# A fused attention, gated mixing and Fourier kernel: inner tiles of the second transform added by VectorE, and three steps moved by a slot

## The chip, the cores and the metric

One Trainium2 chip, one of its cores. The metric is the device time of one execution in microseconds (us); lower is better. All arithmetic is float32, or float32 split into a rounded high part and a low part (fp32r), so that a product takes three matmuls.

## The reference

```python
# attention, per batch (4) and head (8), seq 576, head_dim 64
scores = scale * np.matmul(q, k.transpose(0, 1, 3, 2))
thresh = np.max(scores, axis=-1, keepdims=True) - tau
scores = np.where(scores >= thresh, scores, -1000000000.0)
attn = softmax(scores); out = np.matmul(attn, v)
# gated mixing, x is (4, 576, 512)
xk = mu_k * x + (1.0 - mu_k) * x_prev;  xr = mu_r * x + (1.0 - mu_r) * x_prev
k = np.maximum(xk @ w_k, 0.0);  v = k * k @ w_v;  r = sigmoid(xr @ w_r);  x = r * v
# Fourier mixing, then a normalised MLP (512 -> 2048 -> 512)
mixed = np.real(fft(fft(x, axis=1), axis=2));  u = x + mixed
un = (u - mean) / np.sqrt(var + 1e-06)
out = u + np.maximum(un @ w_ch1, 0.0) @ w_ch2
```

## The kernel before, in words

Each engine runs a list of its own, written out by hand; only semaphores tie the lists together. The lists are built from a common table of **slots**. Slot n handles query tile n of the attention: there are 36 tiles in a batch (4 pairs of heads, 9 tiles in a pair) and 144 in all. Beside the attention of batch b+1 runs the dense work of batch b, placed by slot numbers counted from the start of batch b+1. "Slot 7" below means slot 7 of such a batch.

In a slot the engines do, in this order:
- TensorE (PE): `qk(n)` scores of tile n; `transpose_probs(n-3)`; `pv(n-4)`; then the dense work of the slot.
- VectorE (DVE): `row_max(n)` (L1249) which reads the scores from PSUM; `mask(n-1)` (L1263); then the dense work, the older batch's first. From the second batch on the scores have one PSUM buffer, so `qk(n)` waits until `row_max(n-1)` is done (L731).
- ScalarE (ACT): `exp(n)` (L998, L999); dense work; `copy_units(n-2)` (L1008) copies transposed probabilities out of PSUM; `copy_head(n-5)` (L1021, L1026) copies a finished head from PSUM to `x_att`, in slots where a head ended.
- GpSimd (POOL): `split_step` (L541 to L563) splits keys and queries of a coming head into high and low parts: step 1 `k_hi`, step 2 the high part of `q_hl`, step 3 `k_lo`, step 4 the low part of `q_hl`; the first steps of a pair are spread over three slots by `second_head` and `next_head` (steps 3 and 4 in one slot). Then the dense work.
- SyncE (SP) issues the DMAs.

The dense work of a batch, by slot: x, the transposes of `x_att` (L845, L850) at 2, 2, 4, 5, 5 (`X_AT`), copied out by DVE and ACT (L1336, L1090); mixing, 16 steps at `MIX_AT`: ACT scales `xT` (L1070), DVE adds (L1282), ACT rounds to `mix_h` one slot later (L1084), POOL subtracts to `mix_l` in that slot (L614); then the matmul groups "r" (slots 8 to 11, four groups; the first needs `mix_l` of steps 0 to 3), "k" and "v" from slot 12 on by `slot_of`; the first "k" group needs `mix_l` of steps 4 to 7. Then the two transforms: fold, "y", and "u". The five u groups stand at slots 39, 39, 42, 42, 43 (`U_AT`), so in slots 3, 3, 6, 6, 7 of the next batch. From u groups 0 to 3 ACT and DVE form `diff[0..1]` and `summ[0..1]` (L1147, L1396, L1397), and POOL adds them into the four tiles of `x2T` (`add_dft`, L645 and L646, two instructions a tile): tile 0 in slot 6, tiles 1 and 2 in slot 7, tile 3 in slot 8, after ACT copied one row of u group 4 (L1153, L1154). The sum is stored by DMA (L465). Mixing step 4 rounds into memory that the adds still read, so ACT waits for all of them (L1078).

In the last batch (from slot 144 on) there is no attention beside the dense work. After it comes the MLP, five chunks of columns.

Of the kernel before, what the change touches and what calls it, by code (L numbers as in the profile page):

```python
# [92 lines left out]
X_AT = [2, 2, 4, 5, 5]  # L93
MIX_AT = [3, 4, 5, 6, 7, 8, 9, 10, 12, 13, 14, 15, 17, 18, 19, 20]
FOLD_AT = [32, 35]
# [10 lines left out]
def alone(d):  # L106
    return d == B - 1
# [6 lines left out]
def slot_of(d, stage, c, i, part=0):  # L114

    if (stage, c) == ("r", 0):
        return 8 + i
    done = 0
    for other in stages(d)[1:]:
        if other == (stage, c):  # L120
            return 12 + (done + i * PARTS[stage] + part) * 23 // 36
        done += GROUPS[other[0]] * PARTS[other[0]]
# [42 lines left out]
def build(nc, qT, kT, v, tau, mu_k, mu_r, w_k, w_v, w_r, w_1, w_2, dft_d, dft_odd, dft_s, ident_in, cd_scr, odd_scr, cs_scr, u_scr, out):  # L165
    ctx = ExitStack()
    with ctx:
# [205 lines left out]
        head0_k_hi, head0_q_hi, head0_first, head0_k_low, qk_hi, k_rounded = [sem(n) for n in ("head0_k_hi", "head0_q_hi", "head0_first", "head0_k_low", "qk_hi", "k_rounded")]  # L373
        k_split, qk_split, v_padded = sem("k_split"), sem("qk_split"), sem("v_padded")
        scores_ready, max_ready, thr_ready = sem("scores_ready"), sem("max_ready"), sem("thr_ready")
# [37 lines left out]
        with nc.Block() as block:  # L413

            @block.sync
            def _(sp):
# [35 lines left out]
                def store_u(d):  # L452
                    if d == B - 1:
                        yield X_AT[4] + 1
                        sp.wait_ge(tx_ready, B * 5)
                        load_u(0, 0)
                        load_u(1, 1)
                        load_w2(0)
                    yield U_AT[4] + 2
                    if d == B - 1:  # L460
                        load_w2(1)
                        sp.wait_ge(dft_ready, B * 5)
                        load_w2(2)
                    sp.wait_ge(u_part, d * 3 + 3)
                    sp.dma_start(u_scr[:, :, d * S:d * S + S], x2T[:, :, :]).then_inc(u_stored, 16)  # L465
# [69 lines left out]
            def _(pool):  # L535
# [7 lines left out]
                def split_step(pair, p, step):  # L543
                    n = pair * 2 + p
                    if step == 1:
                        pool.wait_ge(qk_in[p], 64 * pair + 64)
                        if pair > 0:

                            pool.wait_ge(scores_ready, pair * TILES_PAIR if p else pair * TILES_PAIR - FULL)
                        rounded(k_hi[:, p, :], k_raw[:, p, :]).then_inc(k_rounded, 1)  # L550
                    if step == 2:
                        rounded(q_hl[:, p, :], q_raw[:, p, :]).then_inc(qk_hi, 1)
                    if step == 3:
                        pool.wait_ge(k_rounded, n)
                        nc.gpsimd.tensor_tensor(k_lo[:, p, :], k_raw[:, p, :], k_hi[:, p, :].bitcast(F32), ALU.subtract).then_inc(k_split, 1)
                    if step == 4:
                        if n == 1:

                            pool.wait_ge(qk_split, 1)

                        pool.wait_ge(k_split, n)
                        pool.wait_ge(qk_hi, n)
                        nc.gpsimd.tensor_tensor(q_hl[64:128, p, :], q_raw[64:128, p, :], q_hl[64:128, p, :].bitcast(F32), ALU.subtract).then_inc(qk_split, 1)  # L563
                        pool.wait_ge(qk_split, n + 1)

# [50 lines left out]
                def dense(d):  # L616
# [374 lines left out]
            def _(act):  # L991
# [65 lines left out]
                def mixing(d):  # L1057

                    for i in range(16):
# [26 lines left out]
                def dense(d):  # L1086
# [134 lines left out]
            def _(dve):  # L1221
# [108 lines left out]
                def dense(d):  # L1330
# [61 lines left out]
                    for pr in range(2):  # L1392
# [143 lines left out]
```

## Time and profile before

| what | value |
|---|---|
| runs | 1119.99 us median of 3 (1119.54 to 1124.38) |
| profiled execution | 1123.25 us |
| its span, first to last instruction | 1121.4 us |
| mean granted TensorE clock | 0.983 |
| busy share PE, DVE, ACT, POOL | 96%, 50%, 46%, 37% |
| MLP, by the span | from about 711 us to the end |

Read the table as one engine that is nearly always busy and three that are not: PE's idle time over the whole span is some 41 us, and the profiled execution is 3.3 us longer than the median run.

### The profile page before, as it was taken

To read this page: it belongs to the slowest core of one execution; us is meant where nothing else is said; L and a number is where in the kernel's file an instruction comes from. 1 tells how busy PE (TensorE), PEld (TensorE's weight loads), DVE (VectorE), ACT (ScalarE), POOL (GpSimd) and SP (SyncE) were. 2 spreads that over 40 slices of the span, in tenths; PEclk is the share of its full clock that TensorE was granted. 3 is DMA by queue.
4 is the path that set the end of the run, shared out by engine and by line. 5 is a ranking of instruction groups with operands and counts; after the bars stand their busy time and mean duration, and the time that the engine had idled before them with its cause. 6 is when DMAs were issued, how large, how long until landed. Compare 5 with 4: busy or idle time off the path is not lost.

```text
span 1121.4 us, 18463 instructions
## 1 busy us (share of the span) xinstructions
PE 1080.7 (96%) x7088; PEld 1013.4 (90%) x7088; DVE 557.5 (50%) x1081; ACT 513.2 (46%) x1250; POOL 419.5 (37%) x360
## 2 busy tenths in 40 slices
PE   6999999999999999899998997999999999999998
PEld 6989999998899998899996996888888888888998
DVE  6998764565564565564562557344214214123211
ACT  4989875646775646776643733221111011011110
POOL 3897663533763533762512364350111111111000
PEclk9999999999999999999997997999999999999999
DMA  8635111041211141301112107300200200100000
GB/s 229 181 98 169 41 39 34 26 145 45 88 34 34 32 141 42 95 26 34 39 65 105 44 1 289 117 1 1 68 1 1 68 1 1 67 1 1 35 1 33
DMA packets 37251, 69.30 MB, mean 62 GB/s; under 512 B 4134, under 2 KB 18604, under 8 KB 36140
## 3 DMA queue, kind: packets, MB, share of 16 engines
q1 hardware_dynamic: 36860, 67.80, 19.1%
q8 instruction: 56, 0.92, 0.4%
q10 hardware_dynamic: 304, 0.33, 0.1%
q14 instruction: 31, 0.25, 0.1%
HBM read 55.84 MB, written 12.28 MB: 61 GB/s over the span
## 4 chain that ended last, share of the span: by engine, by line
PE 81%; DVE 7%; POOL 5%; issue 3%; ACT 3%; DMA 0%; ACTq 0%; DVEq 0%; POOLq 0%
PE PB L714 20%; PE PB L716 19%; PE PB L715 19%; PE PB L771 9%; PE PB L741 6%; PE PB L754 5%; DVE probs L1263 2%; DVE neg_s L1249 1%; POOL mix_l L614 1%; POOL x2T L645 1%; POOL q_hl L563 1%; POOL fold_l L637 1%; ACT exps L999 1%; POOL x2T L646 1%; DVE pair_sum L1406 1%
## 5 line engine op out<-in xcount | busy, mean ns | idle before, releaser
L1207 ACT ACTIVATE h_hi<-PB 128x464 fp32r<-128x464 f32 (+1 forms) x80 | 44.5, 556 | 335.6 <-PE PB L716 335.6
L1438 DVE SCALAR_TENSOR_TENSOR h_lo<-PB,h_hi 128x464 fp32r<-128x464 f32 (+1 forms) x80 | 51.0, 638 | 264.0 <-ACT h_hi L1207 264.0
L771 PE MATMUL PB<-v_sb,probsT 128*128 128x64 f32 (+1 forms) x1440 | 178.7, 272 | 0.0
L771 PEld LDWEIGHTS PB<-v_sb,probsT 128*128 128x128 f32 x1440 | 173.7, 193 | 0.0
L1008 ACT ACTIVATE probsT<-PB 128x384 f32<-128x384 f32 (+1 forms) x288 | 109.6, 433 | 83.7 <-PE PB L754 82.7
L1263 DVE SCALAR_TENSOR_TENSOR probs<-neg_s,thresh,exps 128x576 f32<-128x576 f32 x144 | 146.7, 1019 | 0.2 <-PE PB L754 0.2
L1249 DVE TENSOR_SCALAR_CACHE_REDUCE neg_s<-PB,taus 128x576 f32<-128x576 f32 x144 | 117.1, 813 | 39.6 <-PE PB L741 35.2
L714 PE MATMUL PB<-un_h,w1h 128*128 128x464 f32 (+1 forms) x320 | 121.7, 380 | 0.0
L716 PE MATMUL PB<-un_h,w1l 128*128 128x464 f32 (+1 forms) x320 | 118.9, 371 | 0.0
L715 PE MATMUL PB<-h_lo,w2h 128*128 128x464 f32 (+1 forms) x320 | 118.8, 371 | 0.0
L714 PE MATMUL PB<-h_hi,w2h 128*128 128x464 f32 (+1 forms) x320 | 118.8, 371 | 0.0
L716 PE MATMUL PB<-h_hi,w2l 128*128 128x464 f32 (+1 forms) x320 | 118.8, 371 | 0.0
L715 PE MATMUL PB<-un_l,w1h 128*128 128x464 f32 (+1 forms) x320 | 118.5, 370 | 0.0
L999 ACT ACTIVATE exps<-neg_s,negmax 128x576 f32<-128x576 f32 x144 | 111.1, 772 | 0.0
L614 POOL TENSOR_TENSOR mix_l<-mix_v,mix_h 128x288 fp32r<-128x288 f32 x64 | 54.0, 844 | 149.0 <-ACT mix_h L1084 117.5
L754 PE MATMUL PB<-ident,probs 128*128 128x128 f32 x720 | 104.5, 277 | 4.8 <-ACT probsT L1008 4.0
L754 PEld LDWEIGHTS PB<-ident,probs 128*128 128x128 f32 x720 | 87.1, 142 | 6.8 <-issue 5.7
L741 PE MATMUL PB<-k_hi,q_hl 128*128 128x288 f32 x320 | 75.5, 317 | 10.9 <-DVE q_hl L1234 8.7
L629 POOL TENSOR_TENSOR k_sql<-k_sq,k_sqh 128x288 fp32r<-128x288 f32 x56 | 48.5, 870 | 89.6 <-DVE k_sq L1349 89.6
L1282 DVE SCALAR_TENSOR_TENSOR mix_v<-xT,mus,mix_v 128x288 f32<-128x288 f32 x64 | 45.0, 703 | 71.5 <-ACT mix_v L1070 71.0
L714 PE MATMUL PB<-mix_h,wkh 128*128 128x288 f32 x256 | 78.8, 308 | 0.9 <-POOL mix_l L614 0.7
L714 PE MATMUL PB<-k_sqh,wvh 128*128 128x288 f32 x256 | 78.7, 308 | 0.4 <-POOL k_sql L629 0.3
(154 smaller groups left out, 2412.2 us busy)
## 6 DMA issues: line engine op xcount, KB each, us to landing
q_raw<-qT_dram SPq DMA_DIRECT2D x62, 160.0 KB, 3.2
k_raw<-kT_dram SPq DMA_DIRECT2D x64, 144.0 KB, 3.2
w_raw<-w_dram SPq DMA_DIRECT2D x8, 1024.0 KB, 9.6
cs<-cs_scr SPq DMA_DIRECT2D x4, 1740.0 KB, 7.8
u_scr<-x2T SPq DMA_DIRECT2D x4, 1152.0 KB, 5.1
cd<-cd_scr SPq DMA_DIRECT2D x4, 1032.0 KB
v_sb<-v_dram SPq DMA_DIRECT2D x16, 256.0 KB, 3.0
u_in<-u_scr SPq DMA_DIRECT2D x4, 928.0 KB, 6.4
```

The source lines that it names most:

```text
L614: nc.gpsimd.tensor_tensor(mix_l[kind][:, dt, :], mix_v[:, i % 2, :], mix_h[kind][:, dt, :].bitcast(F32), ALU.subtract).then_inc(mixl_ready, 1)
L714: nc.tensor.matmul(o, ah, rh, start=start, stop=False)
L715: nc.tensor.matmul(o, ah, rl, start=False, stop=False)
L716: return nc.tensor.matmul(o, al, rh, start=False, stop=stop)
L741: last = nc.tensor.matmul(scores(n)[:, half, :], q_hl[:, h, i * P128:(i + 1) * P128], kk[:, h, half * HALF:half * HALF + HALF], start=h == ...
L754: last = nc.tensor.transpose(bank(4 + unit % 2)[:, (kt - k0) * P128:(kt - k0 + 1) * P128], probs[:, n % 2, kt * P128:(kt + 1) * P128], ide ...
L771: last = nc.tensor.matmul(bank(6 + p)[:, i * DH:i * DH + width], probsT[:, n % 2, kt * P128:(kt + 1) * P128], v_sb[:, kt, pair % 2, p * DH ...
L999: nc.scalar.activation(exps[:, n % 2, :], neg_s[:, n % 2, :], ACT.Exp, bias=negmax[:, col:col + 1], scale=-1.0).then_inc(exp_ready, 1)
L1008: nc.scalar.activation(probsT[:, n % 2, k0 * P128:k1 * P128], bank(4 + unit % 2)[:, 0:(k1 - k0) * P128], ACT.Copy).then_inc(unit_copied, 1)
L1249: nc.vector.tensor_scalar(neg_s[:, n % 2, :].rearrange("p (a n) -> p a n", a=2), scores(n), taus[:, 2:3], None, ALU.mult, ALU.min, accum_o ...
L1263: nc.vector.scalar_tensor_tensor(probs[:, n % 2, 0:S], neg_s[:, n % 2, :], thresh[:, col:col + 1], exps[:, n % 2, :], ALU.is_le, ALU.mult, ...
L1438: nc.vector.scalar_tensor_tensor(h_lo[:, ft % 3, 0:w], bank(4 + ft % 3)[:, 0:w], 0.0, h_hi[:, ft % 3, 0:w].bitcast(F32), ALU.max, ALU.subt ...
```

## The change

Four edits, and the semaphores that go with them.
1. The adds into tiles 1 and 2 of `x2T` are taken from POOL (slot 7) and put on DVE (slot 6), right behind `summ[1]`. The semaphore `u_part` becomes two: `u_outer` (tiles 0 and 3, POOL) and `u_inner` (tiles 1 and 2, DVE). Tiles 0 and 3 stay on POOL at their slots.
2. Of the splits, the low part of `q_hl` comes before `k_lo`, and in the slot of the high part of `q_hl`; `k_lo` has the third slot to itself.
3. Mixing steps 4 to 7 are one slot later (8 to 11), and the groups from "k" on are spread over 22 slots from slot 13 instead of 23 from slot 12.
4. `copy_head` copies a head one slot sooner (`n - 4`).

```diff
-MIX_AT = [3, 4, 5, 6, 7, 8, 9, 10, 12, 13, 14, 15, 17, 18, 19, 20]
+MIX_AT = [3, 4, 5, 6, 8, 9, 10, 11, 12, 13, 14, 15, 17, 18, 19, 20]
...
-            return 12 + (done + i * PARTS[stage] + part) * 23 // 36
+            return 13 + (done + i * PARTS[stage] + part) * 22 // 36
...
+        def add_dft(engine, tile, near, far):
+            engine.tensor_tensor(x2T[:, tile, 0:NYQ], x2T[:, tile, 0:NYQ], near[:, 0:NYQ], ALU.add)
+            return engine.tensor_tensor(x2T[:, tile, NYQ:S], x2T[:, tile, NYQ:S], far[:, NYQ - 2:0:-1], ALU.add)
...
                     if step == 3:
-                        pool.wait_ge(k_rounded, n)
-                        nc.gpsimd.tensor_tensor(k_lo[:, p, :], k_raw[:, p, :], k_hi[:, p, :].bitcast(F32), ALU.subtract).then_inc(k_split, 1)
+                        pool.wait_ge(qk_hi, n)
+                        nc.gpsimd.tensor_tensor(q_hl[64:128, p, :], q_raw[64:128, p, :], q_hl[64:128, p, :].bitcast(F32), ALU.subtract).then_inc(q_low, 1)
+                        pool.wait_ge(q_low, n)
                     if step == 4:
...
-                        nc.gpsimd.tensor_tensor(q_hl[64:128, p, :], q_raw[64:128, p, :], q_hl[64:128, p, :].bitcast(F32), ALU.subtract).then_inc(qk_split, 1)
-                        pool.wait_ge(qk_split, n + 1)
+                        pool.wait_ge(k_rounded, n)
+                        nc.gpsimd.tensor_tensor(k_lo[:, p, :], k_raw[:, p, :], k_hi[:, p, :].bitcast(F32), ALU.subtract).then_inc(qk_split, 1)
...
                     yield U_AT[2]
                     pool.wait_ge(ab_ready, d * 2 + 1)
-                    add_dft(0, diff[0], summ[0]).then_inc(u_part, 1)
-                    yield U_AT[4]
-                    pool.wait_ge(ab_ready, d * 2 + 2)
-                    add_dft(1, diff[1], summ[1])
-                    add_dft(2, summ[1], diff[1]).then_inc(u_part, 1)
+                    add_dft(nc.gpsimd, 0, diff[0], summ[0]).then_inc(u_outer, 1)
                     yield U_AT[4] + 1
                     pool.wait_ge(row_copied, d + 1)
-                    add_dft(3, summ[0], diff[0]).then_inc(u_part, 1)
+                    add_dft(nc.gpsimd, 3, summ[0], diff[0]).then_inc(u_outer, 1)
...
-                second_head = {0: (1,), 1: (2,), 2: (3, 4)}
-                next_head = {5: (1,), 6: (2,), 7: (3, 4)}
+                second_head = {0: (1,), 1: (2, 3), 2: (4,)}
+                next_head = {5: (1,), 6: (2, 3), 7: (4,)}
...
-                            act.wait_ge(u_part, d * 3)
+                            act.wait_ge(u_inner, d)
+                            act.wait_ge(u_outer, d * 2)
...
-                    if 0 <= n - 5 < TILES and (n - 5) % TILES_PAIR in (TAIL, TILES_PAIR - 1):
-                        copy_head(n - 5)
+                    if 0 <= n - 4 < TILES and (n - 4) % TILES_PAIR in (TAIL, TILES_PAIR - 1):
+                        copy_head(n - 4)
...
                         nc.vector.tensor_tensor(summ[pr][:, :], cos, q_cp[pr][:, :], ALU.add).then_inc(ab_ready, 1)
+                    dve.wait_ge(ab_ready, d * 2 + 2)
+                    add_dft(nc.vector, 1, diff[1], summ[1])
+                    add_dft(nc.vector, 2, summ[1], diff[1]).then_inc(u_inner, 1)
```

The other waits on `u_part` (the store, L465; `square(1)`; the row copy; the third `h_lo` of the MLP) become waits on `u_outer`, `u_inner` or both, for the same adds.

**POOL, slots 7 and 8**, as they stand in its list before (`x2T` rows are the adds, `mix_l_84` is step 3 of mixing, which the first "r" group needs, `mix_l_86` is step 4):

```order
L555 TENSOR_TENSOR k_lo<-k_raw,k_hi 128x576
L563 TENSOR_TENSOR q_hl<-q_raw,q_hl 64x640
L645 TENSOR_TENSOR x2T<-x2T,diff_108 128x289
L646 TENSOR_TENSOR x2T<-x2T,summ_110 128x287
L645 TENSOR_TENSOR x2T<-x2T,summ_110 128x289
L646 TENSOR_TENSOR x2T<-x2T,diff_108 128x287
L614 TENSOR_TENSOR mix_l_84<-mix_v,mix_h_83 128x288
L645 TENSOR_TENSOR x2T<-x2T,summ_109 128x289
L646 TENSOR_TENSOR x2T<-x2T,diff_107 128x287
L614 TENSOR_TENSOR mix_l_86<-mix_v,mix_h_85 128x288
```

And POOL from slot 6 to the end of slot 8 in the change:

```order
L546 TENSOR_SCALAR q_hl<-q_raw 128x640
L560 TENSOR_TENSOR q_hl<-q_raw,q_hl 64x640
L408 TENSOR_TENSOR x2T<-x2T,diff_107 128x289
L409 TENSOR_TENSOR x2T<-x2T,summ_109 128x287
L617 TENSOR_TENSOR mix_l_84<-mix_v,mix_h_83 128x288
L567 TENSOR_TENSOR k_lo<-k_raw,k_hi 128x576
L617 TENSOR_TENSOR mix_l_84<-mix_v,mix_h_83 128x288
L408 TENSOR_TENSOR x2T<-x2T,summ_109 128x289
L409 TENSOR_TENSOR x2T<-x2T,diff_107 128x287
```

Five instructions left slot 7 ahead of `mix_l` of step 3: the low part of `q_hl`, now in slot 6, and the four adds. Only `k_lo` is still ahead of it there.

**DVE, slots 6 and 7**, in the change (L1393 and L1394 are `diff[1]` and `summ[1]`, L1279 is mixing step 3, L1246 is `row_max(7)`):

```order
L1393 TENSOR_TENSOR diff_108<-PB,q_cp_106 128x290
L1394 TENSOR_TENSOR summ_110<-PB,q_cp_106 128x290
L408 TENSOR_TENSOR x2T<-x2T,diff_108 128x289
L409 TENSOR_TENSOR x2T<-x2T,summ_110 128x287
L408 TENSOR_TENSOR x2T<-x2T,summ_110 128x289
L409 TENSOR_TENSOR x2T<-x2T,diff_108 128x287
L1279 SCALAR_TENSOR_TENSOR mix_v<-xT,mus,mix_v 128x288
L1246 TENSOR_SCALAR neg_s,negmax<-PB,taus 128x576
```

Before, mixing step 3 and `row_max(7)` followed `summ[1]` directly; now four adds stand between.

**ACT, slots 3 and 4**, before, from `copy_units(1)` on (L1084 and L1070 are the rounding of step 0 and the scaling of step 1):

```order
L1008 ACTIVATE probsT<-PB 128x256
L998 ACTIVATE thresh<-negmax,taus 128x1
L999 ACTIVATE exps<-neg_s,negmax 128x576
L1084 ACTIVATE mix_h_83<-mix_v 128x288
L1070 ACTIVATE mix_v<-xT,omus 128x288
L1008 ACTIVATE probsT<-PB 128x384
L1008 ACTIVATE probsT<-PB 128x256
L1021 ACTIVATE x_att<-PB,rowinv 128x64 x4
```

And in the change:

```order
L1003 ACTIVATE probsT<-PB 128x256
L1016 ACTIVATE x_att<-PB,rowinv 128x64 x4
L993 ACTIVATE thresh<-negmax,taus 128x1
L994 ACTIVATE exps<-neg_s,negmax 128x576
L1080 ACTIVATE mix_h_83<-mix_v 128x288
L1065 ACTIVATE mix_v<-xT,omus 128x288
L1003 ACTIVATE probsT<-PB 128x384
L1003 ACTIVATE probsT<-PB 128x256
```

The head copy moved ahead of `exp(4)` and of both mixing instructions.

## Rows read from the trace of the kernel before

**Rows 1.** Page, part 1: busy time, share, instructions of each engine.
```profile
PE 1080.7 (96%) x7088; PEld 1013.4 (90%) x7088; DVE 557.5 (50%) x1081; ACT 513.2 (46%) x1250; POOL 419.5 (37%) x360
```

**Rows 2.** Stretches: length, busy PE, PEld, DVE, ACT, POOL, clock, DMA share, GB/s.
```profile
160.00:250.00 90.00, 89.87 (x724) 89.53 (x722) 51.78 (x122) 51.48 (x136) 36.95 (x36) 1.00 0.21 64
```

**Rows 3.** Waits of PE, 128 to 720 us: total us, times, longest.
```profile
PE PB L714 <- POOL mix_l L614: 6.2, 4, 2.7
```

**Rows 4.** Timeline, slots 7 and 8, second batch: start, us, instruction, idle before.
```profile
281.00 1.64 POOL L555 TENSOR_TENSOR k_lo<-k_raw,k_hi 128x576 fp32r<-128x576 f32 x1
...
282.72 1.95 POOL L563 TENSOR_TENSOR q_hl<-q_raw,q_hl 64x640 fp32r<-64x640 f32 x1
...
283.81 0.42 ACT L1084 ACTIVATE mix_h<-mix_v 128x288 fp32r<-128x288 f32 x1
...
284.75 1.14 POOL L645 TENSOR_TENSOR x2T<-x2T,diff 128x289 f32<-128x289 f32 x1
...
288.62 0.79 POOL L614 TENSOR_TENSOR mix_l<-mix_v,mix_h 128x288 fp32r<-128x288 f32 x1
...
289.46 0.61 PE L714 MATMUL PB<-mix_h,wrh 128*128 128x288 f32 x1 [2.71 <-POOL mix_l L614]
```

**Rows 5.** Timeline of PE: next "r" group, second batch; same two places, third batch.
```profile
293.54 0.38 PE L714 MATMUL PB<-mix_h,wrh 128*128 128x288 f32 x1
...
457.40 0.41 PE L714 MATMUL PB<-mix_h,wrh 128*128 128x288 f32 x1 [2.71 <-POOL mix_l L614]
...
460.02 0.38 PE L714 MATMUL PB<-mix_h,wrh 128*128 128x288 f32 x1
```

**Rows 6.** Stretches, columns as in rows 2: after the wait; hand-over to the last batch.
```profile
288.00:291.00 3.00, 1.54 (x6) 1.54 (x7) 0.00 (x0) 0.00 (x0) 2.92 (x4) 0.70 0.18 47
...
590.00:640.00 50.00, 44.82 (x276) 40.08 (x275) 20.51 (x41) 25.96 (x65) 16.70 (x20) 0.83 0.23 84
```

**Rows 7.** Timeline, slots 6 to 8, second batch: DVE, and the next scores on PE.
```profile
279.88 0.46 DVE L1396 TENSOR_TENSOR diff<-PB,q_cp 128x290 f32<-128x290 f32 x1 [1.96 <-ACT q_cp L1147]
...
280.25 0.45 DVE L1397 TENSOR_TENSOR summ<-PB,q_cp 128x290 f32<-128x290 f32 x1
...
280.63 0.73 DVE L1282 SCALAR_TENSOR_TENSOR mix_v<-xT,mus,mix_v 128x288 f32<-128x288 f32 x1
...
281.28 0.80 DVE L1249 TENSOR_SCALAR_CACHE_REDUCE neg_s<-PB,taus 128x576 f32<-128x576 f32 x1
...
283.11 0.53 PE L741 MATMUL PB<-k_hi,q_hl 128*128 128x288 f32 x2
```

**Rows 8.** Timeline: DVE behind POOL (slot 8), and POOL behind DVE (last fold).
```profile
285.87 1.39 DVE L1263 SCALAR_TENSOR_TENSOR probs<-neg_s,thresh,exps 128x576 f32<-128x576 f32 x1
...
688.50 3.56 POOL L637 TENSOR_TENSOR fold_l<-fold_v,fold_h 128x289 fp32r<-128x289 f32 x2 [2.41 <-ACT fold_h L1132]
688.66 2.07 DVE L1320 TENSOR_TENSOR cent<-cent,rstd 128x1856 f32<-128x1856 f32 x1
```

**Rows 9.** Timeline, slots 4 to 6, second batch: head copy, row maximum, PE.
```profile
271.93 0.94 ACT L1021 ACTIVATE x_att<-PB,rowinv 128x64 f32<-128x64 f32 x4
...
272.59 0.80 DVE L1249 TENSOR_SCALAR_CACHE_REDUCE neg_s<-PB,taus 128x576 f32<-128x576 f32 x1
...
273.00 0.63 PE L845 MATMUL PB<-ident,x_att 128*128 128x128 f32 x4 [0.55 <-ACT x_att L1021]
...
273.95 0.53 PE L741 MATMUL PB<-k_hi,q_hl 128*128 128x288 f32 x2
```

**Rows 10.** Timeline: third batch, slots 10 to 12; last batch, first "k"; MLP.
```profile
467.60 0.74 DVE L1282 SCALAR_TENSOR_TENSOR mix_v<-xT,mus,mix_v 128x288 f32<-128x288 f32 x1 [2.27 <-ACT mix_v L1070]
...
469.29 0.43 PE L741 MATMUL PB<-k_hi,q_hl 128*128 128x288 f32 x2
...
626.51 0.40 PE L714 MATMUL PB<-mix_h,wkh 128*128 128x288 f32 x1 [0.54 <-POOL mix_l L614]
...
713.83 0.64 DVE L1438 SCALAR_TENSOR_TENSOR h_lo<-PB,h_hi 128x464 fp32r<-128x464 f32 x1 [3.63 <-ACT h_hi L1207]
```

More of the change, by code:

```diff
@@ L373, in build @@
         head0_k_hi, head0_q_hi, head0_first, head0_k_low, qk_hi, k_rounded = [sem(n) for n in ("head0_k_hi", "head0_q_hi", "head0_first", "head0_k_low", "qk_hi", "k_rounded")]
-        k_split, qk_split, v_padded = sem("k_split"), sem("qk_split"), sem("v_padded")
+        q_low, qk_split, v_padded = sem("q_low"), sem("qk_split"), sem("v_padded")
         scores_ready, max_ready, thr_ready = sem("scores_ready"), sem("max_ready"), sem("thr_ready")
@@ L386, in build @@
         dft_ready, qcp_ready, ab_ready, row_copied = [sem(n) for n in ("dft_r", "qcp_r", "ab_r", "row_copied")]
-        u_part, u_stored = sem("u_part"), sem("u_stored")
+        u_outer, u_inner, u_stored = sem("u_outer"), sem("u_inner"), sem("u_stored")
         w1_in = [sem(f"w1_in{i}") for i in range(4)]
@@ L463, in store_u @@
                         load_w2(2)
-                    sp.wait_ge(u_part, d * 3 + 3)
+                    sp.wait_ge(u_inner, d + 1)
+                    sp.wait_ge(u_outer, d * 2 + 2)
                     sp.dma_start(u_scr[:, :, d * S:d * S + S], x2T[:, :, :]).then_inc(u_stored, 16)
@@ L559, in split_step @@
                             pool.wait_ge(qk_split, 1)
-                        pool.wait_ge(k_split, n)
-                        pool.wait_ge(qk_hi, n)
-                        nc.gpsimd.tensor_tensor(q_hl[64:128, p, :], q_raw[64:128, p, :], q_hl[64:128, p, :].bitcast(F32), ALU.subtract).then_inc(qk_split, 1)
-                        pool.wait_ge(qk_split, n + 1)
+                        pool.wait_ge(k_rounded, n)
+                        nc.gpsimd.tensor_tensor(k_lo[:, p, :], k_raw[:, p, :], k_hi[:, p, :].bitcast(F32), ALU.subtract).then_inc(qk_split, 1)
                 def wr_low(t):
@@ L642, in dense @@
                             pool.wait_ge(foldl_ready, d * 5 + 3)
-                    def add_dft(tile, near, far):
-                        nc.gpsimd.tensor_tensor(x2T[:, tile, 0:NYQ], x2T[:, tile, 0:NYQ], near[:, 0:NYQ], ALU.add)
-                        return nc.gpsimd.tensor_tensor(x2T[:, tile, NYQ:S], x2T[:, tile, NYQ:S], far[:, NYQ - 2:0:-1], ALU.add)
                     yield U_AT[2]
                     pool.wait_ge(ab_ready, d * 2 + 1)
-                    add_dft(0, diff[0], summ[0]).then_inc(u_part, 1)
-                    yield U_AT[4]
-                    pool.wait_ge(ab_ready, d * 2 + 2)
-                    add_dft(1, diff[1], summ[1])
-                    add_dft(2, summ[1], diff[1]).then_inc(u_part, 1)
+                    add_dft(nc.gpsimd, 0, diff[0], summ[0]).then_inc(u_outer, 1)
                     yield U_AT[4] + 1
                     pool.wait_ge(row_copied, d + 1)
-                    add_dft(3, summ[0], diff[0]).then_inc(u_part, 1)
+                    add_dft(nc.gpsimd, 3, summ[0], diff[0]).then_inc(u_outer, 1)
                 def add_tiles(src, done, c):
@@ L1149, in dense @@
                     act.wait_ge(dft_ready, d * 5 + 5)
-                    act.wait_ge(u_part, d * 3 + 1)
+                    act.wait_ge(u_outer, d * 2 + 1)
                     row = ring(d, "u", 0, 4)[0:1, 0:FS]
@@ L1158, in square @@
                     if c == 1:
-                        act.wait_ge(u_part, 3 * B)
+                        act.wait_ge(u_inner, B)
+                        act.wait_ge(u_outer, 2 * B)
                     w = width_of(c)
@@ L1435, in chunk @@
                         if first and ft == 2:
-                            dve.wait_ge(u_part, 3 * B)
+                            dve.wait_ge(u_outer, 2 * B)
                         nc.vector.scalar_tensor_tensor(h_lo[:, ft % 3, 0:w], bank(4 + ft % 3)[:, 0:w], 0.0, h_hi[:, ft % 3, 0:w].bitcast(F32),
```

## The prediction

> **What bounds the kernel now.** I read the busy shares first, then stretches, then what PE waits for, then the timeline at those waits. PE is busy 1080.7 of 1121.4 us, the other three engines half the time or less [rows 1]. In the steady part of a batch PE is busy 89.87 of 90 us at full clock [rows 2], so nothing that only relieves another engine can show there. What can be won is PE's idle time at the hand-over from one batch to the next. There the waits of PE name `mix_l`: 6.2 us in four waits, the longest 2.71 [rows 3]. The timeline shows why [rows 4]: in slot 7 POOL works through `k_lo`, the low part of `q_hl` (1.64 and 1.95 us) and four adds into `x2T` (from 284.75 to 288.6) before it comes to the `mix_l` that the first "r" group needs as its last operand; PE stands still for 2.71 us until 289.46. The third batch shows the same wait, 2.71 us again [rows 5]. The other two waits are 0.54 us in the last batch [rows 10] and, by difference, 0.2 us.
>
> A second cost hangs on the first wait. After it the granted clock falls: 0.70 on average in the next 3 us, so part of them at 1.2 GHz instead of 2.4 [rows 6]. From the late matmul to the next "r" group takes 293.54 - 289.46 = 4.08 us in the second batch, 460.02 - 457.40 = 2.62 in the third, with the same work [rows 5]: 1.46 us more. The third batch had an equal wait and no fall, so this part comes by chance and not in every execution.
>
> **The change, part by part**, against the profiled execution's own 1123.25 us.
>
> *The wait for `mix_l` goes: -5.4.* Five instructions leave POOL's slot 7, and only `k_lo` stays ahead. They took 1.95 us plus the four adds, from 284.75 to 288.6. In the new list `mix_l` follows ScalarE's `mix_h`. That one ended at 284.23, 2.15 us after `row_max(7)` [rows 4, 7], so `mix_l` (0.79) can end about 3.0 us after the row maximum. PE comes to the matmuls that need it 289.46 - 2.71 - 283.11 = 3.64 us after the start of `qk(8)`, which itself waits for that row maximum. So it is in time by some 0.6 us. Gain 2 x 2.71. Where the clock fell after it, 1.4 more.
>
> *The adds go to DVE, ahead of `row_max(7)`: +1.5.* They stand behind `summ[1]` and ahead of mixing step 3 and the row maximum, for which `qk(8)` waits. Before, `row_max(7)` ended at 281.28 + 0.80 = 282.1 and PE came to `qk(8)` at 283.11 [rows 7]: 1.0 us of slack. An add of this size on DVE costs the 0.37 us between the starts of `diff` and `summ` [rows 7] (its span is 0.45), four of them 1.5 us. They must also wait for POOL where both read SBUF: the mask at 285.87 took 1.39 us beside POOL's adds, 0.6 more than the row maximum of the same width [rows 8, 7]. Here POOL has `mix_l` of step 2 in hand, about 0.4 us left of it; against that, mixing step 3, whose 0.73 us [rows 7] held part of the same wait, gives back some 0.2 (both estimates). So 1.5 + 0.4 - 0.2 - 1.0 = 0.7, taken as 0.75, twice. Bounds each: 0.3 (nothing in hand) and 2.2. The upper one lets `k_lo` (1.64) in ahead of the adds. Whether it gets in between them is told by the fold of the last batch: POOL's two `fold_l` took 3.56 us, since the first waited from 688.50 until DVE's whole run of instructions, the 2.07 us one at 688.66 the last of it, was over [rows 8]. A run of DVE instructions is held together, so I stay near the low bound. The Trainium skill (SBUF — State Buffer, "Who interferes with whom") has whoever starts first keep the shared ports for one whole instruction while the other is fully blocked; read strictly, POOL could come in after each add, and the term would be some 3.5 to 4 us in place of 1.5.
>
> *`copy_head` a slot sooner: +0.8.* What it can win is PE's 0.55 us wait for `x_att` in slot 5 [rows 9]. But the copy (0.94 us) now stands ahead of `exp(4)` and mixing step 1 on ACT. DVE waits for that mixing step with the transposed tile and `row_max(5)` queued behind it, so `row_max(5)` ends at 273.39 + 0.93 = 274.3, and PE, which came to `qk(6)` at 273.95, waits for it: about 0.4 later than before in spite of the wait that went. Twice +0.4. Bounds each: -0.55 (DVE catches up) and +0.9. Elsewhere the copy meets no one: nothing waits for a head in mid-batch.
>
> *Splits: 0.* The same four instructions in another order. In the first batch POOL runs them back to back whatever the slot, so nothing moves there; the cover is the 90 us stretch without idle time [rows 2], and if it goes the price is that of one split, 1.95 us, for one batch.
>
> *Mixing steps 4 to 7 and the "k" groups a slot later: +0.7.* The 0.2 us wait of the first "k" group goes. But slot 12 now holds attention alone, so PE comes to `qk(13)` earlier by two dense parts, and DVE has mixing step 7 ahead of `row_max(12)`. Here slack is thin: in slot 11 of the third batch DVE stood 2.27 us waiting for ACT's mixing step, its row maximum came behind that at about 468.3 and ended at 469.1, and PE went on at 469.29 [rows 10]. I take a new wait of 0.3 us in each of three batches, between 0 and 1.0. ACT's long wait for the adds before `mix_h` of step 4 goes, which is what keeps this small.
>
> *Last batch: +0.3.* A part of this hand-over runs at 1.2 GHz (clock 0.83 over 50 us [rows 6]). No row maximum waits behind the adds, but ACT now rounds mixing step 7 behind the fourth gate, and the 0.54 us wait at the first "k" group [rows 10] grows by about 0.3 (0 to 0.9).
>
> *The MLP: 0.* DVE is idle 3.63 us before its first `h_lo` [rows 10], which hides the last four adds (1.5 us).
>
> The sum is -5.4 - 1.4 + 1.5 + 0.8 + 0.7 + 0.3 = -3.5, so 1119.7 for a twin of the profiled execution. That one lies 3.3 us above the median of 1119.99, and I can't see whether the median run had the fall of the clock. Without that term the sum is -2.1, and **my forecast is 1117.9 us**, 0.2% less. A measurement of this kernel can tell about 0.5% (5.6 us) from no change, so this counts as no difference.
>
> **The rivals.**
> *The whole wait is won.* DVE and ACT catch up inside the slots, and the x_att wait goes too: 1119.99 - 5.4 - 1.1 - 0.2 = 1113.3. For it: DVE and ACT are busy half the time [rows 1]. Against it: 1.0 us of slack for 1.5 us of adds.
> *The wait only changes its name.* `k_lo` or a late mixing step gets ahead of the adds and `row_max(7)` is 2.2 us late: 2.9 us more than my sum, 1120.8. The Trainium skill (Perfetto Trace Analysis, "Optimizing Scalar/DVE Operations") says that moving work between the two engines might not help because they share a read port; by that rule this is the case that comes. The 1.39 us mask agrees with it, the 3.56 us of `fold_l` speaks for DVE [rows 8].
> *The clock falls at the new waits.* Three short waits (slots 6, 7 to 8, 13) replace one. At the hand-over to the last batch, which has no attention between its waits, PE was idle 5.2 of 50 us and the clock 0.83 on average: 0.17 x 50 x 2 = 17 us at half clock [rows 6]. With the idle part of them off, that cost about 7 us. Should the hand-over of a batch with attention do so, 1117.9 + 7 = 1124.9 for one, 1131.9 for two. It decides from the point where the new waits of a hand-over sum to more than the 2.71 us of the old one; my terms give 0.4 + 0.75 + 0.3.
> *The clock holds in the last batch*, as its timing shifts: 1117.9 - 7 = 1110.9. The waits there are hardly touched, so this is unlikely.
> *The edits act as no change*: the adds leave, but some other operand of the "r" group is as late (ACT's `mix_h` behind `exp(7)`). I count it with the second rival; its time is the same.
>
> **How the numbers follow.** My own case 0.48, whole wait won 0.18, wait renamed 0.18, clock falls 0.10, clock holds 0.06. Faster by over 0.5% is below 1114.4: most of the second and fifth, and a tail of mine, 0.25. Slower by over 0.5% is above 1125.6: part of the fourth, and what the bounds of all terms add up to (0.09 in all). The rest, 0.66, is within 0.5%. The range from 1111.5 to 1123.5 takes in the bounds of my terms (about -5 and +5) and the first two rivals, and leaves out most of the clock's two.
>
> **What would show it.** In the profile after: PE's wait for `mix_l` of 2.71 us gone in both batches; the adds on DVE at 0.37 to 0.45 us each, the first one longer if POOL was in hand; `qk(8)` 0.5 to 1 us late behind `row_max(7)`; `qk(6)` right behind `row_max(5)`; a short wait at `qk(13)`. I am wrong if `k_lo` runs between the adds, if PE waits nowhere for a row maximum (then the gain is 5 us or more), or if the steady stretch is no longer full.

## The result and the profile after

| kernel | runs | profiled execution, its span | clock |
|---|---|---|---|
| before | 1124.06 us median of 15 (1119.54 to 1129.56) | 1123.25, 1121.4 | 0.983 |
| changed | 1119.13 us median of 15 (1117.46 to 1120.92) | 1120.57, 1118.7 | 0.982 |

The ratio is 0.9964 [0.9949, 0.9978]: 0.4% faster, within the 0.5% that counts as no difference. With more runs the median of the kernel before came out 4 us above the 1119.99 that stood with the three first ones, at the profiled execution's level.

Each run also has a mean granted clock, and it bears on the medians. The 57 runs of the kernel before that stand beside the experiments below have a median clock of 0.980 and a median span of 1121.1 us; the 15 of the changed kernel have 0.982 and 1117.3. As an estimate, (1 - 0.980) x 1121.1 - (1 - 0.982) x 1117.3 = 2.3 us less went to the clock, good to some 1 us, as the clocks are given to three places. And 14 of the 57 have a clock of 0.983 or more, with spans from 1116.7 to 1119.8: the profiled execution of before, 1121.4 at 0.983, is a long one for its clock.

Part 1 of the page and the steady stretch after (columns as in [rows 1, 2]): DVE has 16 instructions more, POOL 16 less, and the stretch is as full as before.
```profile
PE 1081.3 (97%) x7088; PEld 1014.1 (91%) x7088; DVE 570.1 (51%) x1097; ACT 514.0 (46%) x1250; POOL 401.3 (36%) x344
...
160.00:250.00 90.00, 89.54 (x719) 88.99 (x718) 48.32 (x119) 52.05 (x139) 36.87 (x37) 1.00 0.22 65
```
The waits of PE after, 128 to 720 us (total, times, longest). It answers to [rows 3]; of the kernel before one more row of that view is given, the second below.
```profile
PE PB L736 <- DVE neg_s L1246: 4.7, 4, 2.1
PE PB L845 <- DVE xT L1333: 1.8, 3, 1.0
...
PE PB L709 <- POOL mix_l L617: 1.0, 1, 1.0
```
```profile
PE PB L714 <- POOL mix_l L614: 6.2, 4, 2.7
PE PB L845 <- ACT x_att L1021: 2.7, 3, 1.6
```
The wait for `mix_l` is gone from the hand-overs of the second and third batch; the 1.0 us that is left is in the last batch. In its place stands one for `neg_s`, the row maximum: 8.9 us of waits became 7.5, and 7.9 with a new one of 0.4 in the last batch, for an `xT` that ACT copies out. The timeline of slots 6 to 8 in the second batch shows how ([rows 4, 7] of before):
```profile
277.51 0.45 DVE L1394 TENSOR_TENSOR summ<-PB,q_cp 128x290 f32<-128x290 f32 x1
...
277.85 0.79 POOL L617 TENSOR_TENSOR mix_l<-mix_v,mix_h 128x288 fp32r<-128x288 f32 x1
278.00 0.97 DVE L408 TENSOR_TENSOR x2T<-x2T,diff 128x289 f32<-128x289 f32 x1
278.61 1.63 POOL L567 TENSOR_TENSOR k_lo<-k_raw,k_hi 128x576 fp32r<-128x576 f32 x1
...
278.88 1.67 DVE L409 TENSOR_TENSOR x2T<-x2T,summ 128x287 f32<-128x287 f32 x1
...
280.48 0.45 DVE L408 TENSOR_TENSOR x2T<-x2T,summ 128x289 f32<-128x289 f32 x1
...
280.85 0.45 DVE L409 TENSOR_TENSOR x2T<-x2T,diff 128x287 f32<-128x287 f32 x1
281.21 0.51 DVE L1279 SCALAR_TENSOR_TENSOR mix_v<-xT,mus,mix_v 128x288 f32<-128x288 f32 x1
281.64 0.81 DVE L1246 TENSOR_SCALAR_CACHE_REDUCE neg_s<-PB,taus 128x576 f32<-128x576 f32 x1
...
282.51 0.61 PE L736 MATMUL PB<-k_hi,q_hl 128*128 128x288 f32 x2 [2.08 <-DVE neg_s L1246]
...
284.45 0.80 POOL L617 TENSOR_TENSOR mix_l<-mix_v,mix_h 128x288 fp32r<-128x288 f32 x1 [4.21 <-ACT mix_h L1080]
```
The first add stands behind POOL's `mix_l` (0.97 us in place of 0.45). While it runs, POOL comes to `k_lo`, and `k_lo` gets in ahead of the second add, which is held for 1.67 us. The row maximum starts 281.64 - 277.51 = 4.13 us after `summ`; before it was 281.28 - 280.25 = 1.03 [rows 7], so the four adds delay it by 3.1 us, where 1.5 + 0.4 - 0.2 had been worked out. PE waits 2.08 us. The third batch repeats the three durations, 1.63, 1.67 and 2.08, to the hundredth:
```profile
446.14 1.63 POOL L567 TENSOR_TENSOR k_lo<-k_raw,k_hi 128x576 fp32r<-128x576 f32 x1
446.42 1.67 DVE L409 TENSOR_TENSOR x2T<-x2T,summ 128x287 f32<-128x287 f32 x1
...
450.04 0.85 PE L736 MATMUL PB<-k_hi,q_hl 128*128 128x288 f32 x2 [2.08 <-DVE neg_s L1246]
```
And behind both waits the clock falls (stretches, columns as in [rows 2]; the last row answers to [rows 6]):
```profile
280.00:284.00 4.00, 1.92 (x10) 1.67 (x10) 3.56 (x9) 1.51 (x5) 0.24 (x1) 0.85 0.54 147
284.00:288.00 4.00, 4.00 (x26) 4.00 (x25) 2.05 (x5) 2.37 (x7) 3.55 (x4) 0.72 0.03 9
448.00:452.00 4.00, 1.96 (x8) 1.94 (x9) 3.32 (x9) 1.88 (x5) 0.02 (x1) 0.76 0.58 155
452.00:456.00 4.00, 4.00 (x29) 4.00 (x28) 2.01 (x5) 2.28 (x6) 3.65 (x4) 0.82 0.01 3
590.00:640.00 50.00, 44.65 (x274) 40.09 (x274) 22.51 (x45) 27.37 (x69) 14.25 (x17) 0.83 0.23 84
```
A clock of 0.85 and 0.72 over 4 us each is (0.15 + 0.28) x 4 = 1.7 us lost, and 1.7 again in the third batch. PE's own times agree: from `qk(8)` to the first "r" matmul takes 286.34 - 282.51 = 3.83 us here, and 3.83 in the third batch, but 283.51 - 281.30 = 2.21 in the run below in which the clock held. The profiled execution of before had one such fall, this one has two.

### The profile page after: what moved, and what is told of

The parts are those of the page before. It is cut to its first block, busy times and chain, and to the rows that moved or that the text cites. A ratio compares the mean times of both kernels' runs of the same rounds, so it can differ in the third digit from the quotient of the medians.

```text
span 1118.7 us, 18441 instructions
## 1 busy us (share of the span) xinstructions
PE 1081.3 (97%) x7088; PEld 1014.1 (91%) x7088; DVE 570.1 (51%) x1097; ACT 514.0 (46%) x1250; POOL 401.3 (36%) x344
## 4 chain that ended last, share of the span: by engine, by line
PE 87%; DVE 7%; ACT 3%; issue 2%; POOL 1%; DMA 0%; ACTq 0%; DVEq 0%; POOLq 0%
PE PB L709 21%; PE PB L711 20%; PE PB L710 20%; PE PB L766 11%; PE PB L736 7%; PE PB L749 6%; DVE probs L1260 2%; DVE neg_s L1246 1%; POOL fold_l L640 1%; DVE pair_sum L1406 1%; DVE rowinv L1270 0%; ACT mix_v L1065 0%; DMA taus<-tau_dram 0%; ACT exps L994 0%; DVE x2T L409 0%
## 5 line engine op out<-in xcount | busy, mean ns | idle before, releaser
L1260 DVE SCALAR_TENSOR_TENSOR probs<-neg_s,thresh,exps 128x576 f32<-128x576 f32 x144 | 151.2, 1050 | 0.7 <-PE PB L749 0.7
L1246 DVE TENSOR_SCALAR_CACHE_REDUCE neg_s<-PB,taus 128x576 f32<-128x576 f32 x144 | 117.2, 814 | 51.8 <-PE PB L736 47.6
L1279 DVE SCALAR_TENSOR_TENSOR mix_v<-xT,mus,mix_v 128x288 f32<-128x288 f32 x64 | 48.7, 761 | 55.2 <-ACT mix_v L1065 55.1
```

The lines of the kernel that those rows point to most:

```text
L1246: nc.vector.tensor_scalar(neg_s[:, n % 2, :].rearrange("p (a n) -> p a n", a=2), scores(n), taus[:, 2:3], None, ALU.mult, ALU.min, accum_o ...
L1260: nc.vector.scalar_tensor_tensor(probs[:, n % 2, 0:S], neg_s[:, n % 2, :], thresh[:, col:col + 1], exps[:, n % 2, :], ALU.is_le, ALU.mult, ...
```

## The experiments

The theory after the result: the new order of the splits carries the gain, and the adds on VectorE give part of it back, since `k_lo` gets in among them, the row maximum is late, and the clock falls behind the wait. Each ratio below is to the kernel before, run beside it (medians there 1122.49 to 1123.3). Edits are against the changed kernel unless said otherwise.

### Where the adds stand

**Adds of tiles 1 and 2 back on POOL**, all other edits kept:
```diff
+                    yield U_AT[4]
+                    pool.wait_ge(ab_ready, d * 2 + 2)
+                    add_dft(nc.gpsimd, 1, diff[1], summ[1])
+                    add_dft(nc.gpsimd, 2, summ[1], diff[1]).then_inc(u_inner, 1)
...
-                    dve.wait_ge(ab_ready, d * 2 + 2)
-                    add_dft(nc.vector, 1, diff[1], summ[1])
-                    add_dft(nc.vector, 2, summ[1], diff[1]).then_inc(u_inner, 1)
```


> The changed kernel with the adds of tiles 1 and 2 back on POOL in slot 7; the splits stay as changed. It tells which edit removed the wait for mix_l. Theory (both were needed: the low part of q_hl is 1.95 us of the 2.71, the adds the rest): the wait for mix_l of step 3 is 0.7 to 1.3 us in both hand-overs, no wait for a row maximum at qk(8), no fall of the clock there, time 1116 to 1118, so no worse than the changed kernel. Rival (the adds are what mattered): the wait for mix_l is over 2 us and the time 1120 to 1122.

Measured: 1113.88 us (1113.34 to 1115.17), ratio 0.9925 [0.9904, 0.9946]. Its waits of PE, and the first "r" group of the second batch:
```profile
PE PB L713 <- POOL mix_l L617: 3.7, 3, 1.3
...
PE PB L740 <- DVE neg_s L1250: 0.5, 2, 0.3
```
```profile
284.30 0.40 PE L713 MATMUL PB<-mix_h,wrh 128*128 128x288 f32 x1 [1.34 <-POOL mix_l L617]
```
That is 2 us less than was expected at the least. So the edit that names the change, the adds on VectorE, costs some 5 us where it stands: 1119.1 with it, 1113.9 without, and the intervals of the ratios (0.9949 to 0.9978, 0.9904 to 0.9946) don't overlap. The `mix_l` wait comes back at 1.34 us only, and no fall of the clock follows it.

**The adds a slot later on DVE**, behind `row_max(7)` and `mask(6)`:
```diff
+                   yield U_AT[4]
                    dve.wait_ge(ab_ready, d * 2 + 2)
                    add_dft(nc.vector, 1, diff[1], summ[1])
```


> The changed kernel with the DVE adds one slot later, behind row_max(7) and mask(6) in place of ahead of them. Theory (the 2.1 us wait of qk(8) is the adds ahead of the row maximum, two of them blocked by POOL): that wait goes in both hand-overs, the clock no longer falls behind it, no new wait of over 0.5 us comes, 4 us gained, some 1115. Rival (the time is set by ACT's and DVE's work of the whole hand-over and not by the place of the adds): the wait moves to a later slot, 1118 to 1120.

Measured: 1112.41 us (1111.07 to 1113.94), ratio 0.9912 [0.989, 0.9933]. The longest wait for `neg_s` is 0.4 us, and the time is 2.6 us below the 1115 of the theory. The order on one engine's list decides, not which engine adds: 6.7 us between two places of the same four instructions, one slot apart.

**`k_lo` a slot later, the adds left ahead of the row maximum:**
```diff
-                next_head = {5: (1,), 6: (2, 3), 7: (4,)}
+                next_head = {5: (1,), 6: (2, 3), 8: (4,)}
```


> The changed kernel, with k_lo of the next head given to POOL in slot 8 instead of 7; the four adds stay on VectorE ahead of the row maximum. Lock per instruction (my theory now): with no long POOL instruction at hand the four adds run back to back at 0.45 us, the row maximum of tile 7 ends about 1.6 us sooner and the wait of qk(8), 2.08 us in the changed kernel, falls to 0.3 to 0.9. The clock then falls less at the two hand-overs. Time 1114 to 1117 us. Rival (the adds are in the way by their number, not by the lock): the wait stays above 1.5 us, time 1118 to 1120.

Measured: 1115.81 us (1114.53 to 1117.5), ratio 0.9922 [0.9901, 0.9943]. Timeline:
```profile
278.00 0.97 DVE L408 TENSOR_TENSOR x2T<-x2T,diff 128x289 f32<-128x289 f32 x1
278.90 0.45 DVE L409 TENSOR_TENSOR x2T<-x2T,summ 128x287 f32<-128x287 f32 x1
279.26 0.45 DVE L408 TENSOR_TENSOR x2T<-x2T,summ 128x289 f32<-128x289 f32 x1
279.63 0.45 DVE L409 TENSOR_TENSOR x2T<-x2T,diff 128x287 f32<-128x287 f32 x1
...
280.43 0.81 DVE L1246 TENSOR_SCALAR_CACHE_REDUCE neg_s<-PB,taus 128x576 f32<-128x576 f32 x1
...
281.30 0.53 PE L736 MATMUL PB<-k_hi,q_hl 128*128 128x288 f32 x2 [0.87 <-DVE neg_s L1246]
```
This is the sharpest of them. Up to the first add the timeline reads as in the changed kernel; with `k_lo` away the second add takes 0.45 in place of 1.67 us, and the wait is 0.87 in place of 2.08: 1.22 us of the one are 1.21 us of the other. The clock stays at full speed in these three stretches:
```profile
280.00:284.00 4.00, 3.13 (x26) 2.90 (x25) 3.55 (x10) 2.72 (x9) 0.76 (x1) 1.00 0.00 0
284.00:288.00 4.00, 3.56 (x30) 3.32 (x29) 2.31 (x4) 2.92 (x8) 4.00 (x5) 1.00 0.20 53
448.00:452.00 4.00, 3.56 (x30) 3.32 (x28) 2.33 (x5) 3.62 (x10) 3.07 (x3) 1.00 0.01 2
```
The 0.87 us that are left are nearly the 0.75 that the prediction gave this wait. The move has a price of its own: `qk(9)` now waits for `k_lo`, 0.44 us in each of the two batches.

### One edit at a time

**The adds alone**: before, with edit 1 only.

> The kernel before with edit 1 alone: only the adds go to DVE; splits, mixing steps and head copy as before. Theory: the low part of q_hl and k_lo are both on POOL while the adds run, so the adds are blocked by up to two POOL instructions and qk(8) waits 2 to 4 us, while the wait for mix_l goes; time 1119 to 1123, no better than the kernel before. Rival (edit 1 brings the whole gain, the rest nothing): about 1118.5 to 1119.5.

Measured: 1124.4 us (1120.65 to 1131.67), ratio 1.0012 [0.9993, 1.0032]. Here `k_lo` and the low part of `q_hl` are both in POOL's slot 7, and both get in:
```profile
277.67 0.63 DVE L408 TENSOR_TENSOR x2T<-x2T,diff 128x289 f32<-128x289 f32 x1
277.94 1.63 POOL L560 TENSOR_TENSOR k_lo<-k_raw,k_hi 128x576 fp32r<-128x576 f32 x1
278.22 1.67 DVE L409 TENSOR_TENSOR x2T<-x2T,summ 128x287 f32<-128x287 f32 x1
279.65 1.63 POOL L568 TENSOR_TENSOR q_hl<-q_raw,q_hl 64x640 fp32r<-64x640 f32 x1
279.80 1.79 DVE L408 TENSOR_TENSOR x2T<-x2T,summ 128x289 f32<-128x289 f32 x1
281.51 0.45 DVE L409 TENSOR_TENSOR x2T<-x2T,diff 128x287 f32<-128x287 f32 x1
...
283.18 0.85 PE L738 MATMUL PB<-k_hi,q_hl 128*128 128x288 f32 x2 [3.08 <-DVE neg_s L1248]
```
The two engines take turns, instruction by instruction. A wait of 3.08 us stands where one of 2.71 stood. The time is 1.4 us above the expected range, and no different from before.

**The order of the splits alone**: before, with edit 2 only.
```diff
-                second_head = {0: (1,), 1: (2,), 2: (3, 4)}
-                next_head = {5: (1,), 6: (2,), 7: (3, 4)}
+                second_head = {0: (1,), 1: (2, 3), 2: (4,)}
+                next_head = {5: (1,), 6: (2, 3), 7: (4,)}
...
```
(The bodies of steps 3 and 4 are exchanged with it, as in the change.)

> The kernel before with the new order of the four splits alone; the adds stay on POOL in slot 7, the mixing slots and the head copy as before. In slot 7 POOL has lost the 1.95 us of q_hl ahead of the adds and mix_l. If it is this that removes the wait, the 2.71 us wait for mix_l falls to 0.8 to 1.3 us in both batches and the clock falls less: 1115 to 1119 us. Rival (the mixing slots do it): the wait stays above 2 us and the time at 1121 to 1124.

Measured: 1113.6 us (1112.9 to 1114.85), ratio 0.9904 [0.9884, 0.9923]. Waits of PE, and two stretches:
```profile
PE PB L713 <- POOL mix_l L617: 1.9, 3, 0.9
```
```profile
280.00:288.00 8.00, 7.53 (x60) 7.13 (x60) 4.14 (x8) 4.80 (x13) 7.37 (x9) 1.00 0.32 91
...
448.00:456.00 8.00, 7.46 (x60) 6.99 (x58) 4.87 (x12) 5.52 (x14) 5.75 (x8) 1.00 0.46 169
```
A better result than expected, and better than the whole change. The 1.95 us of `q_hl` [rows 4] leave POOL's slot 7, the wait for `mix_l` falls by about that in each of the two batches, from 2.71 to 0.47 us (6.2 to 1.9 in all), and the clock no longer falls in the hand-overs. The clock helps to explain how 4.3 us of waits can be worth more than twice as much: its median is 0.986 here and 0.980 in the 17 runs of before beside it, by the same estimate as above some 7 us less lost. The spread shrinks too: those 17 runs lie within 8.2 us, these five within 2.

**The later slots alone**: before, with edit 3 only.

> The kernel before with mixing steps 4 to 7 and the k groups one slot later alone. Step 3, which the first r group waits for, stays in slot 6, and POOL's work of slot 7 loses only mixing step 4, which stood behind it. So the wait for mix_l stays at 2.5 to 2.7 us, and the short wait of the first k group goes: 1121 to 1124 us. Rival (the slots carry the gain): 1115 to 1119 us with the waits below 1.3 us.

Measured: 1124.1 us (1120.02 to 1126.87), ratio 0.9996 [0.9978, 1.0013], with the wait where it was, both times:
```profile
287.97 0.40 PE L715 MATMUL PB<-mix_h,wrh 128*128 128x288 f32 x1 [2.70 <-POOL mix_l L619]
...
456.54 0.40 PE L715 MATMUL PB<-mix_h,wrh 128*128 128x288 f32 x1 [2.70 <-POOL mix_l L619]
```
As expected; the edit is worth nothing by itself. It also shows the wait that the prediction gave it: `qk(13)` waits for the row maximum once in each of three batches, 0.35, 0.33 and 0.34 us.

**The whole change without the new order of the splits.**

> The changed kernel with the splits in the order of the kernel before (q_hl's low part behind k_lo, both in slot 7). POOL then has two long instructions in slot 7, and both can get in between VectorE's adds, as in the run of the adds alone: the wait of qk(8) is 2.5 to 3.1 us, the time 1123 to 1125 us. So without the new order of the splits the change would be worth nothing. Rival (the adds and slots carry a part of the gain): 1119 to 1121 us.

Measured: 1121.73 us (1120.54 to 1123.05), ratio 0.9995 [0.9979, 1.0011], the longest wait for `neg_s` 3.1 us. A little faster than expected, but no different from before: all of the gain came with edit 2.

### The head copy, and the best version

**The head copied as before** (`n - 5`), the rest of the change kept.

> The changed kernel with one edit undone: the head copy is again one slot later. Theory (the head copy a slot sooner costs, since it stands ahead of mixing step 1 on ACT and so ahead of row_max(5) on DVE): the scores of tile 6 of batches 2, 3 and 4 come 0.6 to 0.8 us sooner than in the changed kernel, PE's wait for xT (1.8 us in three) goes, the 0.55 us wait for x_att comes back, and the time is 1 to 2 us below the changed kernel (1117 to 1118). Rival (the copy sooner is what saves time): the time is 1 to 2 us above it (1120 to 1121).

Measured: 1118.66 us (1116.54 to 1123.1), ratio 0.9966 [0.9946, 0.9985]. The wait for `xT` (1.8 us in 3) is gone, one for `x_att` (2.5 us in 3) stands there, and `qk(8)` waits 1.75 in place of 2.08 us. Against the changed kernel (0.9964) nothing can be told.

**Both: adds behind the row maximum, the head copied as before**; run twice, the second time beside the next kernel.

> The run with the adds behind the row maximum (1112.4 us), and the head copied in the slot of the kernel before. If the sooner head copy costs 0.6 to 0.8 us per batch, as its waits for the transposed tile (1.7 us in 3) say, this gives 1110.5 to 1111.5. Rival: the copy only swaps one wait for another (x_att, some 1.4 us in 3), time 1112 to 1113.

> The best kernel so far once more (all of the change but the sooner head copy, with the adds behind the row maximum), beside the run without its later mixing slots on the same chip: 1111.2 us again, within 0.8 us; the difference to the run beside it is what the mixing slots are worth, under 1 us by my theory, 1.5 to 3 us by the rival.

Measured: 1111.17 us (1110.82 to 1114.37), ratio 0.9889 [0.9868, 0.9911]; again: 1112.11 us (1110.48 to 1112.86), ratio 0.9904 [0.9884, 0.9924]. With the head copied sooner it was 1112.41 (0.9912), so the sooner copy is worth nothing or costs up to some 1 us; these runs don't tell. The repeat came out 0.9 us above the first time, a tenth outside what was expected of it.

**Edit 2 and the later adds, nothing else** (slots and head copy as before):
```diff
-MIX_AT = [3, 4, 5, 6, 8, 9, 10, 11, 12, 13, 14, 15, 17, 18, 19, 20]
+MIX_AT = [3, 4, 5, 6, 7, 8, 9, 10, 12, 13, 14, 15, 17, 18, 19, 20]
...
-            return 13 + (done + i * PARTS[stage] + part) * 22 // 36
+            return 12 + (done + i * PARTS[stage] + part) * 23 // 36
...
-                        copy_head(n - 4)
+                        copy_head(n - 5)
...
+                    yield U_AT[4]
                     dve.wait_ge(ab_ready, d * 2 + 2)
```


> The kernel before with two edits: the new order of the splits, and the four adds on VectorE behind the row maximum of tile 7. Mixing slots and head copy as before. If the mixing slots are worth nothing, as their run alone says, this gives what the best run gave: 1110.5 to 1112 us. Rival (the later slots are worth something once the adds are gone): 1112.5 to 1114 us.

Measured: **1110.32 us** (1109.68 to 1114.43), ratio 0.9896 [0.9872, 0.992]. With the smallest change it is as fast as any, 8 to 9 us below the changed kernel. Beside it on the same chip the kernel with the later mixing slots took 1112.11; the intervals of the two ratios overlap, so the slots have no gain, and may cost up to some 2 us. Its hand-overs, on DVE and POOL, and as stretches:
```profile
277.50 1.64 POOL L567 TENSOR_TENSOR k_lo<-k_raw,k_hi 128x576 fp32r<-128x576 f32 x1
277.78 0.81 DVE L1246 TENSOR_SCALAR_CACHE_REDUCE neg_s<-PB,taus 128x576 f32<-128x576 f32 x1
...
278.52 1.24 DVE L1260 SCALAR_TENSOR_TENSOR probs<-neg_s,thresh,exps 128x576 f32<-128x576 f32 x1
...
279.60 0.53 PE L736 MATMUL PB<-k_hi,q_hl 128*128 128x288 f32 x2
...
279.69 0.45 DVE L408 TENSOR_TENSOR x2T<-x2T,diff 128x289 f32<-128x289 f32 x1
```
```profile
276.00:284.00 8.00, 8.00 (x63) 7.67 (x64) 7.63 (x15) 5.87 (x16) 5.83 (x6) 1.00 0.26 78
...
444.00:452.00 8.00, 8.00 (x69) 8.00 (x67) 6.83 (x15) 6.64 (x18) 5.39 (x7) 1.00 0.66 223
```
`k_lo` runs at the same place of POOL's list. But what it meets on DVE is the row maximum, which reads PSUM and takes its usual 0.81 us beside it, and then the mask, which bears the wait (1.24 us, against 0.81 in the changed kernel at 282.38) where nobody needs it soon. The adds come when POOL is done. PE is busy for all of both stretches.

## Why the prediction was right in number, and where its steps failed

**What held.** The bound was PE's waits at the hand-over, and the steady stretch didn't move. `mix_l` was in time, in both batches (-5.4 as worked out, and the 0.2 beside it). From its own base the sum gave 1119.7 for a twin of the profiled execution, and 1119.13 is the median. The forecast of 1117.9 was drawn from the low median of three runs, and was 1.2 us off. The mechanism that came, though, was that of the second rival (the wait changes its name, 1120.8), not mine.

**What was luck.** That the number fits so well is luck. Two costs were forecast some 3 us too low each (`qk(8)`, and the clock between the profiled executions), and the profiled execution of before, the base of the sum, happened to be some 3 us long in its first 36 tiles. The forecast itself stands on a median of three runs that was 4 us low, and on a gain of 2.1 us where the medians of 15 differ by 4.9.

**The step that failed: "A run of DVE instructions is held together, so I stay near the low bound."** The term was 0.75 us a batch; each wait measured 2.08, so +4.2 in place of +1.5. The row read for it, `fold_l` at 3.56 us [rows 8], showed one case in which DVE kept its turn; the runs show POOL taking it in both hand-overs of the changed kernel and twice in one hand-over of the adds alone, and the run with `k_lo` moved gives its price, 1.21 us. The rule that was set against it is that of the Trainium skill (SBUF — State Buffer, "Who interferes with whom"), an exclusive lock for one whole instruction. By it the term was 3.5 to 4 us for the two batches, and the trace agrees, with 4.2 just above. The upper bound of the text (2.2, "lets `k_lo` in ahead of the adds") covered the size.

**The clock: -1.4 forecast, about +1.7 found between the profiled executions.** The fall was counted as gone with its wait. It came back behind the new wait, in both batches (1.7 us each), though that is shorter than the old one: 2.08 against 2.71 us. Over the runs the clock went the other way, by the estimate above 2.3 us less lost, and with its 0.983 the profiled execution of before had lost less than most of its runs (14 of 57 have as much or more). The rival of the clock set its point where the new waits of a hand-over sum to more than 2.71 us. Here they sum to 0.40 + 0.28 + 2.08 = 2.76, and the clock did fall; but with the head copied as before they sum to 0.55 + 1.75 = 2.30 and it fell in one of two, so the sum is not what decides. Nor did its price come, 7 us for a hand-over: it was 1.7.

**Splits: "0, the same four instructions in another order".** The text did count the 1.95 us of `q_hl` among what leaves slot 7, under the wait. But it priced the five instructions as one, and never asked what this one is worth without the other four. It is the change: 9.7 us less alone (1123.3 to 1113.6), where the adds alone give nothing.

**`copy_head`, +0.8:** the new waits in slots 5 and 6 are there:
```profile
270.43 0.46 PE L845 MATMUL PB<-ident,x_att 64*128 64x64 f32 x4 [0.40 <-DVE xT L1333]
...
271.17 0.54 PE L736 MATMUL PB<-k_hi,q_hl 128*128 128x288 f32 x2 [0.28 <-DVE neg_s L1246]
```
`qk(6)` stands right behind the row maximum, as said, 0.28 us late; the 0.40 before it wasn't foreseen. They sum to 0.68, against the 0.55 of [rows 9]. Small and of the right sign; end to end not measurable.

**The "k" groups later, +0.7:** no wait came in slot 13 of the changed kernel, though the slots alone show the forecast one, 0.33 to 0.35 us in three batches. The four waits for `neg_s`, 4.7 us, are 2 x 2.08 and 2 x 0.28. In the last batch the wait for `mix_l` grew from 0.54 to 1.0 us, 0.46 for a forecast 0.3. The MLP hides the last adds, as said: DVE's idle time before its first `h_lo` shrank from 3.63 [rows 10] but is still there.
```profile
711.18 0.64 DVE L1438 SCALAR_TENSOR_TENSOR h_lo<-PB,h_hi 128x464 fp32r<-128x464 f32 x1 [1.41 <-ACT h_hi L1204]
```

So the sum by measured terms, between the two profiled executions, is: `mix_l` -5.6, `qk(8)` +4.2, clock +1.7, head copy +0.3, last batch +0.5 for `mix_l` and -0.2 at its start (1.6 us for `x_att` became 1.0 and 0.4 for the two `xT`), together +0.9, where the span shows -2.7. Of these 3.6 us, 1.4 arise before the first row maximum starts (10.57 us before, 9.21 after), and by the end of the first 36 tiles the changed kernel is 2.1 us further ahead. The second lead was 0.9 to 3.6 us in the other experiments, with 1.8 for the adds alone and 1.1 for the slots alone, whose edits touch nothing there: so much of it goes with the execution and is no term of the change. The five kernels with the sooner head copy have 2.1 to 3.6, the others 0.9 to 2.6; that a part of it is edit 4's isn't shown. Between the medians, the waits (8.9 to 7.9 us) and the clock (2.3 us) make some 3.3 of the 4.9 us, or of the 4.0 that the ratio gives; the rest is open.

## What to carry to other kernels

When several steps leave a slot, price each by itself, with the others left in place: here one of them, a reordering of POOL's list that cost no line of work, is the whole gain. When work goes from POOL to DVE, look at what POOL has in hand at that moment and what waits behind it on DVE; put it behind the instruction on which PE depends, so that the wait falls on one that has slack. And a short wait can cost nearly its own length again through the clock (1.7 us behind 2.08): its share is read from the granted clock of the stretch behind the wait.

## What the hardware showed unexpectedly

- **DVE and POOL alternate by instruction.** In the run of the adds alone two POOL instructions of 1.63 us got in between four adds of 0.45, and the adds behind them took 1.67 and 1.79. POOL had come up 0.28 and 0.15 us ahead of the add it displaced. In the fold of [rows 8] it had come 0.16 us ahead of DVE's next instruction and was yet the one to wait. What decides between the two was not tried and stays open.
- **The clock and the length of a wait.** Each of the thirteen profiled executions (before, after, eleven experiments) has two such hand-overs. Their longest waits there are: ten of 2.08 us or more, of which eight were followed by a stretch at 1.2 GHz; two of 1.74 and 1.75 us, of which the second was; fourteen of 1.34 us or less, of which none was. That is a count, not a bound: of two waits of 2.71 us in the kernel before one had no fall, and of two of 2.70 us in the run of the slots alone as well.
- **The times of the runs go with their granted clock.** Of the 57 runs of the kernel before, twelve with a clock of 0.983 have spans from 1117.8 to 1119.8 us, the 21 with 0.980 from 1120.2 to 1122.6, twelve with 0.979 from 1122.3 to 1124.0, and four with 0.976 some 1126.4. So most of the 10 us of spread between equal runs goes with the clock, and a single run tells little of a change of 5 us.
